# Window attention in groups of four units: sinks of a group turned in one product, bank copies on two engines

## What is computed

```
scores = scale * q @ k.T, kept where is_sink | in_window, else -1e9
a = exp(scores - max) ; a = a / (sum(a) + 1e-09) ; x = a @ v
h = x @ w_in ; x = (h * tanh(softplus(h))) @ w_out
out = sum over e of p[:, e] * (relu(x @ w1[e]) @ w2[e])
```

## Time and profile before

| | us |
|---|---|
| runs (3): lowest, median, highest | 887.83, 887.85, 888.09 |
| profiled execution, its time | 884.6 |
| its span, first to last instruction | 882.8 |
| first scores on TensorE | 7.44 |
| first down product of the first expert layer | 127.26 |

### The profile page before, as it was taken

One profiled execution on the slowest core, in us unless ns is written; L12 is line 12 of the kernel. 1 busy time (PEld: TensorE's weight loads), 2 busy tenths in 40 slices (PEclk: granted clock), 3 DMA queues, 4 the chain that ended last, 5 costly groups with the idle time before them and its releaser, 6 DMA issues.

```text
span 882.8 us, 14223 instructions
## 1 busy us (share of the span) xinstructions
PE 869.5 (98%) x4560; PEld 731.6 (83%) x4560; DVE 603.9 (68%) x1164; ACT 414.7 (47%) x759; POOL 172.0 (19%) x243
## 2 busy tenths in 40 slices
PE   6999999999999999999999999999999999999998
PEld 3566677888888888889999988999988999988997
DVE  5666659988888898986565665655656565565655
ACT  5888866444775454883342243134234323313410
POOL 4855520000110011231220220122022012202100
PEclk9999999999999999999999999999999999999999
DMA  6233344000484000770531551353154144223303
GB/s 242 68 99 109 113 97 97 1 0 1 88 191 103 0 0 0 166 153 16 114 71 44 113 113 26 87 113 61 52 113 103 25 97 113 49 64 65 66 0 143
DMA packets 24229, 70.14 MB, mean 79 GB/s; under 512 B 4224, under 2 KB 5504, under 8 KB 24192
## 3 DMA queue, kind: packets, MB, share of 16 engines
q0 software_dynamic: 10144, 31.72, 19.9%
q1 hardware_dynamic: 13904, 37.58, 12.9%
q10 hardware_dynamic: 144, 0.39, 0.2%
HBM read 34.83 MB, written 3.15 MB: 43 GB/s over the span
## 4 chain that ended last, share of the span: by engine, by line
PE 95%; DVE 2%; ACT 1%; issue 1%; DMA 0%; POOL 0%; DVEq 0%
PE banks L843 30%; PE banks L769 26%; PE banks L740 14%; PE banks L599 13%; PE banks L626 4%; PE banks L645 4%; PE banks L686 3%; PE banks L656 1%; PE banks L697 1%; DMA prm<-params 0%; ACT pool L906 0%; ACT pool L908 0%; DVE g_lo L1427 0%; ACT g_hi L1020 0%; POOL pool L461 0%
## 5 line engine op out<-in xcount | busy, mean ns | idle before, releaser
L1571 DVE SCALAR_TENSOR_TENSOR pool<-banks,p_norm,pool 128x512 f32<-128x512 f32 x180 | 133.6, 749 | 66.7 <-PE banks L843 64.9
L843 PE MATMUL banks<-w_hi,g_lo 128*128 128x512 f32 x384 | 150.6, 392 | 0.0
L843 PE MATMUL banks<-w_lo,g_hi 128*128 128x512 f32 x384 | 150.5, 392 | 0.0
L843 PE MATMUL banks<-w_hi,g_hi 128*128 128x512 f32 x384 | 149.3, 389 | 0.0
L1137 ACT ACTIVATE g_hi<-pool 128x384 fp32r<-128x384 f32 x96 | 50.5, 526 | 190.8 <-DVE pool L1551 139.2
L769 PE MATMUL banks<-x_hi,w_lo 128*128 128x384 f32 x256 | 85.9, 336 | 0.0
L769 PE MATMUL banks<-x_hi,w_hi 128*128 128x384 f32 x256 | 85.9, 335 | 0.0
L769 PE MATMUL banks<-x_lo,w_hi 128*128 128x384 f32 x256 | 85.7, 335 | 0.0
L843 PEld LDWEIGHTS banks<-w_hi,g_lo 128*128 128x128 f32 x384 | 72.1, 188 | 15.2
L843 PEld LDWEIGHTS banks<-w_lo,g_hi 128*128 128x128 f32 x384 | 72.0, 188 | 13.9
L843 PEld LDWEIGHTS banks<-w_hi,g_hi 128*128 128x128 f32 x384 | 72.1, 188 | 13.6
(11 more groups left out here) (135 smaller groups left out, 1777.0 us busy)
## 6 DMA issues: line engine op xcount, KB each, us to landing
w_raw<-weights SPq DMA_DIRECT2D x48, 512.0 KB, 4.3
w_lo<-w_raw POOLq DMA_DIRECT2D x44, 512.0 KB, 5.4
w_lo<-w_sum POOLq DMA_DIRECT2D x15, 384.0 KB, 4.0
pool<-kT SPq DMA_DIRECT2D x8, 400.0 KB, 4.8
pool<-v SPq DMA_DIRECT2D x8, 384.0 KB, 3.0
out<-pool SPq DMA_DIRECT2D x12, 256.0 KB, 2.0
pool<-qT SPq DMA_DIRECT2D x7, 384.0 KB, 4.1
w_lo<-pool POOLq DMA_DIRECT2D x2, 384.0 KB, 5.0
```

Source lines behind the costliest of these rows:

```text
L843: mm = pe.matmul(banks[:, bank, :], g[:, s, f * SUP + at:f * SUP + at + P], w_cols(w, p2 * SLOT + DOWN_AT[f], DM), start=(f == 0 and n == ...
L1571: dve.scalar_tensor_tensor(out=to, in0=d_bank, scalar=share, in1=to, op0=ALU.mult, op1=ALU.add)\
```

## The change

The window case gets streams of its own, `window_attention` on each engine; the case without a window keeps the old one as `full_attention`. Four units, two query tiles with both heads, form a **group** g; there are 6 per `ct`, 3 per half, 24 in all, and 16 of them have sinks (tiles 2 and up).

- TensorE per group: four scores into four banks, values of group g - 2, turns of group g - 1. The two query tiles of a group turn into two fixed banks.
- GpSimd gathers the 4 x 16 sink columns of a group into `sink_prob` (128 x 64). TensorE turns them in one product into 64 rows of the bank that the group's fourth score unit uses, between the turns of the second query tile; VectorE copies 64 x 128.
- The sink values of a query tile are one product over these 64 rows with a matrix of 64 x 128 from `v_sink`, made on the host: of its four bands of 16 rows, one for each unit, only the two of this query tile's heads hold values, each in the 64 columns of its head. There are two such products per group.
- ScalarE copies the bank of the first query tile, VectorE that of the second.
- Inversions are of two units, twice per group, both behind the four maskings of the same group.
- `EARLY` is 5: tiles 0 to 3 are split within attention by ScalarE's two copies (`SPLIT_AT`) and an adding DMA from GpSimd (`ADD_AT`); the subtraction on GpSimd is gone, and so is the zeroing of the sink buffers on VectorE at the start.
- At the end of attention all three up steps stand inside the branch, and so does the whole gate of the first step. ScalarE's and GpSimd's loops over `ct` are written out.

Cut to its core, with blank lines left out:

```
-EARLY = 4
-EARLY_AT = [7, 9, 11, 13, 15, 17, 19, 22]
-SCORE_RING = {True: 4, False: 2}
-SCORE_BANKS = {True: 3, False: 2}
-PROB_RING = {True: 8, False: 3}
-SPLIT_VALUES_AT = 2
-INVERT_LAG = {True: 4, False: 2}
-TOGETHER = {True: 4, False: 2}
-TURN_LAG = {True: 7, False: 2}
-COPY_LAG = {True: 7, False: 2}
-PV_LAG = {True: 9, False: 3}
-TAKE_LAG = {True: 10, False: 4}
-START_UP = [5]
-START_MISH = 5
+EARLY = 5
+FULL_RING, FULL_SCORES, FULL_TOGETHER = 3, 2, 2
+FULL_TURN, FULL_COPY, FULL_PV, FULL_TAKE = 2, 2, 3, 4
+FULL_INVERT = 2
+GROUPS_A = B * QT // 2
+WIDE = 2 * (P + SINKS)
+WINDOW_GROUP = 4 * WIDE + P
+SPLIT_AT = [4 + 2 * n for n in range(2 * (EARLY - 1))]
+ADD_AT = [7 + 4 * n for n in range(EARLY - 1)]
...
+        scores_w = part(SCORES_AT, 4, WIDE)
+        prob_w = part(SCORES_AT + 4 * WIDE, 2, WINDOW_GROUP + P)
...
-        v_sink = part(SINKS_AT, B, P)
-        sink_T = part(SINK_T_AT, 4, 2, P)
+        v_sink = part(SINKS_AT, B, 2 * P)
+        sink_T = part(SINK_T_AT, 2, P)
+        sink_prob = part(SINK_PROB_AT, 2, 4, SINKS)
...
-                return [(f + EARLY + 1, None)] if f + EARLY + 1 < STEPS else []
+                return [(f + EARLY, None)] if f + EARLY < STEPS else []
...
+            def window_attention():
+                width, _, _ = attention_plan(True)
+                for ct in range(CT):
                     for u in range(UNITS):
-                        normalise(ct, u)
+                        if u % 2 == 0:
+                            pl.wait_ge(den_ready, ct * (UNITS // 2) + u // 2 + 1)
+                        w = width[u // 2 % QT]
+                        normalise(window_prob(u, w), u, w)
+                        group = ct * GROUPS_A + u // 4
+                        if u % 4 == 3 and w == WIDE - SINKS:
+                            pl.wait_ge(prob_ready, ct * UNITS + u + 1)
+                            sinks = prob_w[:, group % 2, P:P + 4 * WIDE].rearrange("p (a b) -> p a b", a=4)[:, :, 0:SINKS]
+                            pl.tensor_copy(sink_prob[:, group % 2, :, :], sinks).then_inc(sinks_ready, 1)
+                        if u % 4 == 3 and group in ADD_AT:
+                            k = ADD_AT.index(group)
+                            add_raw(k, k, k + 1)
...
+                def scores(ct, g):
+                    for u in range(4 * g, 4 * g + 4):
+                        inputs_ready(ct, u)
+                        if not early(ct, u, 4):
+                            pe.wait_ge(masked, ct * UNITS + u - 3)
+                        copied = sinks_before(g - 1) if g >= 1 else sinks_before(GROUPS_A - 1) - SINK_GROUPS
+                        if u % 4 == 3 and (not isinstance(ct, int) or copied > 0):
+                            pe.wait_ge(sink_out, ct * SINK_GROUPS + copied)
+                        score_of(u, u // (2 * QT), u // 2 % QT, banks[:, UP_BANK + u % 4, :], segments)
+                def turn(ct, g, scored_units):
+                    for n in range(2):
+                        u = 4 * g + 2 * n
+                        pe.wait_ge(prob_ready, ct * UNITS + u + 2)
+                        if not early(ct, g, 1):
+                            pe.wait_ge((first_copied, second_copied)[n], ct * GROUPS_A + g)
+                        with_sinks = n == 1 and g % (QT // 2) > 0
+                        if with_sinks:
+                            pe.wait_ge(sinks_ready, ct * SINK_GROUPS + sinks_before(g) + 1)
+                            pe.wait_ge(masked, scored_units)
+                        for h in range(2):
+                            if h == 1 and with_sinks:
+                                sinks = sink_prob[:, g % 2, :, :].rearrange("p a b -> p (a b)")
+                                pe.transpose(sink_bank, sinks, ident[:, :])
+                            for k, (col, _) in enumerate(blocks[u // 2 % QT]):
+                                mm = pe.transpose(banks[:, TURN_BANK + n, P * (2 * h + k):P * (2 * h + k) + P],
+                                                  window_prob(u + h, WIDE)[:, col:col + P], ident[:, :])
+                        mm.then_inc(turned, 1)
+                def values(ct, g):
+                    b = g // (QT // 2)
+                    sinks = g % (QT // 2) > 0
+                    def sink_values(n):
+                        j = 2 * (g % (QT // 2)) + n
+                        mm = pe.matmul(banks[:, OUT_BANK + j // 4, P * (j % 4):P * (j % 4) + P],
+                                       v_sink[0:4 * SINKS, b, P * n:P * n + P], sink_T[0:4 * SINKS, g % 2, :],
+                                       start=(n == 1), stop=(n == 0), skip_group_check=True)
+                        if n == 0:
+                            mm.then_inc(pv_done, 2)
+                    for n in range(2):
+                        j = 2 * (g % (QT // 2)) + n
+                        if j == 0:
+                            pe.wait_ge(v_in[b], 32 * ct + 32)
+                        if j % 4 == 0:
+                            pe.wait_ge(x_lo_done, ct * (2 * B) + 2 * b + j // 4 + 1)
+                        pe.wait_ge((first_copied, second_copied)[n], ct * GROUPS_A + g + 1)
+                        out_bank, column = OUT_BANK + j // 4, slice(P * (j % 4), P * (j % 4) + P)
+                        slot = 2 * (g % 2) + n
+                        for k, (_, kt) in enumerate(blocks[j]):
+                            for h in range(2):
+                                mm = pe.matmul(banks[D * h:D * h + D, out_bank, column], v_pair[:, b, kt, D * h:D * h + D],
+                                               prob_T[:, slot, P * (2 * h + k):P * (2 * h + k) + P],
+                                               start=(k == 0 and not (sinks and n == 1)),
+                                               stop=(k == len(blocks[j]) - 1 and not (sinks and n == 0)),
+                                               skip_group_check=sinks)
+                        if n == 1 or not sinks:
+                            mm.then_inc(pv_done, 2)
+                        if sinks and n == 0:
+                            pe.wait_ge(sink_out, ct * SINK_GROUPS + sinks_before(g) + 1)
+                            sink_values(0)
+                            sink_values(1)
+                def period(ct, g, before):
+                    scores(ct, g)
+                    if at := group_at(ct, g, 2, before):
+                        values(*at)
+                    if at := group_at(ct, g, 1, before):
+                        turn(*at, ct * UNITS + 4 * g + 4)
+                for g in range(GROUPS_A):
+                    period(0, g, False)
+                with pe.Fori(1, CT) as ct:
+                    for g in range(GROUPS_A):
+                        period(ct, g, True)
+                start_up(0)
+                values(CT - 1, GROUPS_A - 2)
+                turn(CT - 1, GROUPS_A - 1, CT * UNITS)
+                start_up(1)
+                values(CT - 1, GROUPS_A - 1)
+                start_up(2)
...
+                def copy_first(ct, g):
+                    j = 2 * (g % (QT // 2))
+                    act.wait_ge(turned, 2 * (ct * GROUPS_A + g) + 1)
+                    two_units = [t.rearrange("p (u n) -> p u n", u=2)[:, :, 0:P * len(blocks[j])]
+                                 for t in (prob_T[:, 2 * (g % 2), :], banks[:, TURN_BANK, :])]
+                    act.activation(*two_units, ACT.Copy).then_inc(first_copied, 1)
...
+                for ct in range(CT):
+                    for g in range(GROUPS_A):
+                        for u in range(4 * g, 4 * g + 4):
+                            if u % 4 == 0 and ct * GROUPS_A + g >= 2:
+                                act.wait_ge(turned, 2 * (ct * GROUPS_A + g) - 2)
+                            w = width[u // 2 % QT]
+                            exponent(ct, u, window_prob(u, w), scores_w[:, u % 4, 0:w], u % 4)
+                        if at := group_at(ct, g, 1, ct > 0):
+                            copy_first(*at)
+                        if at := group_at(ct, g, 2, ct > 0):
+                            take_after(*at)
+                        if ct * GROUPS_A + g in SPLIT_AT:
+                            n = SPLIT_AT.index(ct * GROUPS_A + g)
+                            if n % 2 == 0:
+                                split_tile_hi(0, n // 2, None)
+                            else:
+                                split_tile_neg(n // 2)
+                split_tile_hi(0, EARLY - 1, None)
+                split_tile_neg(EARLY - 1)
+                exponential(0)
+                take_after(CT - 1, GROUPS_A - 2)
+                reciprocal(0)
+                copy_first(CT - 1, GROUPS_A - 1)
+                take_after(CT - 1, GROUPS_A - 1)
...
+                def copy_second(ct, g):
+                    j = 2 * (g % (QT // 2)) + 1
+                    dve.wait_ge(turned, 2 * (ct * GROUPS_A + g) + 2)
+                    if g % (QT // 2):
+                        dve.tensor_copy(sink_T[0:4 * SINKS, g % 2, :], sink_bank)\
```

(38 more changed lines are left out.)

467 lines of the change are left out of this document (192 added, 275 removed).

## The result

The changed kernel takes **876.77 us** (median of 4 runs, 875.9 to 877.4) against 887.84, a ratio of 0.9885 with a 95% interval of 0.9855 to 0.9915. The profiled executions differ less: 884.6 before and 877.4 after (spans 882.8 and 875.6). That one had been forecast at 878.1. So there are two questions: whether the 7.2 us in the traces went where the prediction says, and where the other 4 come from.

What follows compares the result with a forecast made beforehand. TensorE bounds before; after, a VectorE-ScalarE loop of 11.40 us a half: 10.7 + 7 x 11.40 + 16.8 = 107.3 against 119.8, gain 12.5 less 24 waits of 0.25 for GpSimd, 6.5; predicted 881.3 us, range 874.5 to 887.5.

Steps and rivals of the forecast that it cites:

- forecast at 878.1: Profiled execution of the changed kernel: 884.6 us less a gain of 6.5; the median was put 3.25 higher, at 881.3.
- the loop that the other engines now close per group: Steady attention: VectorE, ScalarE, VectorE per group, 3.59 + 3.78 + 4.03 = 11.40 us a half, above TensorE's 10.6.
- the point where the two meet: Rival: TensorE and the loop hinder each other, as at the sink copy; halves 0.3 to 0.6 us longer, 884 to 886; chance 0.13.
- offset between a profiled execution and the median: Last step: the median of the runs lies 3.25 us above the profiled execution, carried over to the changed kernel.

## What to carry to other kernels

When work is regrouped so that the bound engine changes kind less often, write down the loop that the other engines now close per group, and add the point where the two meet: here 11.2 and 11.5 gave 12.0, and moving one copy ahead of one inversion gave 0.4 of it back. A small instruction that used to stand far behind its data costs nothing; put next to its data in a loop, two of them in each group cost 3.5 us. And before an offset between a profiled execution and the median is carried over, find out what it consists of.

## What was unexpected of the hardware

- The place of a branch in the program is worth several us on each side: no gap at the exit against 3.95 us on ScalarE and 1.42 on TensorE, and 6.5 us at the entry. The page "Advanced Engine Details and Errata" of the Trainium skill, section "Control Flow Timing", has a branch at about 51 ns; no run here times a branch alone, and the gaps are some 30 to 130 times that, so the branch by itself does not account for them.
- TensorE's slow start lasted until 16.0 to 24.7 us where it began near 7.5, and differed between two traces of one kernel. The granted clock in their windows stands at 1.00 throughout, the 2.4 GHz level, while the matmuls take 1.7 times their later time, so these rows do not show it:

```profile
20.00:24.00 4.00, 4.00 (x21) 1.00 0.04 16
24.00:28.00 4.00, 4.00 (x38) 1.00 0.02 4
```

These are TensorE's windows of 4 us in the trace of the kernel before with one reciprocal: 21 instructions, then 38, most of them at the full pace.

- An instruction of 128x2 elements waits until GpSimd's running multiplications end (0.51 and 0.65 us for 0.17), and up to 1.00 with the second copy on ScalarE; a reciprocal of the same size in its place took 0.153 to 0.167 in all 48 cases.
